# Strided and local attention with a rational MLP: row shape of the casts in memory, and queue order, PSUM banks and engine choices drawn anew

## The reference

```
scores = scale * q @ k^T                       # per batch and head
mask_local   = (rel >= 0) & (rel < 32)         # heads 0 to 3, rel = row - column
mask_strided = (rel >= 0) & (col % 32 == row % 32)   # heads 4 to 7
attn = exp(scores - max) / (sum + 1e-9), masked
x = (attn @ v), heads side by side             # 4608 x 512
h = x @ w_in                                   # 512 x 2048
P = a0 + a1*h + a2*h^2 + a3*h^3
Q = 1 + |b0|*|h| + |b1|*h^2
out = (P / (Q + 1e-6)) @ w_out                 # 2048 x 512
```

## Time and profile before

| | |
|---|---|
| three runs | 356.49, 356.37, 352.88 us; median 356.37 us |
| profiled execution | 355.32 us, of which the traced span is 353.5 us |
| busy in the span | PE 92%, DVE 91%, ACT 87%, POOL 21% |
| mean granted TensorE clock | 0.981 of full speed |

### The profile page before, as it was taken

One profiled execution on the slowest core, in us unless ns is written; L12 is line 12 of the kernel. 1 busy time (PEld: TensorE's weight loads), 2 busy tenths in 40 slices (PEclk: granted clock), 3 DMA queues, 4 the chain that ended last, 5 costly groups with the idle time before them and its releaser, 6 DMA issues.

```text
span 353.5 us, 9960 instructions
## 1 busy us (share of the span) xinstructions
PE 325.6 (92%) x4502; PEld 169.3 (48%) x4548; DVE 322.5 (91%) x282; ACT 307.1 (87%) x299; POOL 75.6 (21%) x112
## 2 busy tenths in 40 slices
PE   4979989999889998999999699999999999999796
PEld 1547667454444454455444354454444444444342
DVE  6573389999999999999999799999999999999995
ACT  6775389799998599999998798899999999999880
POOL 8980007060037043038003240000000000000000
PEclk9995799999999999999999999999999999999999
DMA  8999949999999999899699959510410011200203
GB/s 118 188 156 199 201 95 132 191 182 157 190 192 162 201 208 148 207 214 164 94 229 160 118 123 218 122 63 23 97 23 32 0 49 42 89 0 32 89 30 119
DMA packets 94314, 44.68 MB, mean 126 GB/s; under 512 B 79424, under 2 KB 87360, under 8 KB 93888
## 3 DMA queue, kind: packets, MB, share of 16 engines
q0 software_dynamic: 30528, 18.23, 42.1%
q1 hardware_dynamic: 63200, 25.69, 34.9%
q10 hardware_dynamic: 544, 0.13, 0.2%
HBM read 36.87 MB, written 16.52 MB: 151 GB/s over the span
## 4 chain that ended last, share of the span: by engine, by line
PE 60%; DVE 29%; ACT 6%; issue 4%; DVEq 0%
PE ps L1098 23%; PE ps L1168 22%; DVE h L1151 4%; DVE u L1126 4%; DVE z L1143 3%; DVE z L1147 3%; PE ps L683 3%; DVE u L1123 2%; DVE z L1140 2%; PE ps L1258 2%; DVE z L1149 2%; DVE z L1145 2%; ACT h L314 2%; DVE qkT L314 1%; PE ps L876 1%
## 5 line engine op out<-in xcount | busy, mean ns | idle before, releaser
L1168 PE MATMUL ps<-Wout,h 128*128 128x512 bf16 x543 | 129.2, 379 | 8.7 <-issue 5.9
L1098 PE MATMUL ps<-XT,Win 128*128 128x512 bf16 (+1 forms) x627 | 131.7, 361 | 4.9 <-issue 2.9
L1098 PEld LDWEIGHTS ps<-XT,Win 128*128 128x128 bf16 x640 | 61.5, 99 | 68.7 <-issue 4.0
L314 ACT ACTIVATE h<-ps 128x1024 bf16<-128x1024 f32 (+1 forms) x80 | 71.8, 958 | 16.6 <-PE ps L1098 16.6
L1168 PEld LDWEIGHTS ps<-Wout,h 128*128 128x128 bf16 x576 | 52.9, 98 | 63.7 <-issue 3.5
L1131 ACT ACTIVATE u<-u 128x4096 bf16<-128x4096 bf16 (+2 forms) x22 | 66.2, 3009 | 0.4 <-DVE u L1126 0.4
L1136 ACT ACTIVATE u<-u 128x4096 bf16<-128x4096 bf16 (+2 forms) x22 | 66.2, 3010 | 0.1
L1126 DVE TENSOR_TENSOR u<-u,z 128x4096 bf16<-128x4096 bf16 (+2 forms) x21 | 41.6, 1980 | 0.4
L1151 DVE TENSOR_TENSOR h<-z,u 128x4096 bf16<-128x4096 bf16 (+2 forms) x21 | 41.4, 1978 | 0.3
L1147 DVE TENSOR_TENSOR z<-z,h 128x4096 bf16<-128x4096 bf16 (+2 forms) x21 | 41.4, 1977 | 0.1
L1143 DVE TENSOR_TENSOR z<-z,h 128x4096 bf16<-128x4096 bf16 (+2 forms) x21 | 41.4, 1977 | 0.1
(11 more groups left out here) (106 smaller groups left out, 274.8 us busy)
## 6 DMA issues: line engine op xcount, KB each, us to landing
out_dram<-os SPq DMA_DIRECT2D x32, 256.0 KB, 2.5
qk<-in_k_dram POOLq DMA_DIRECT2D x12, 288.0 KB, 6.0
qk<-in_q_dram POOLq DMA_DIRECT2D x12, 288.0 KB, 6.1
Win<-in_moe_w_in_dram POOLq DMA_DIRECT2D x2, 1024.0 KB, 16.0
Wout<-in_moe_w_out_dram POOLq DMA_DIRECT2D x2, 1024.0 KB, 23.7
vS<-in_v_dram POOLq DMA_DIRECT2D x28, 72.0 KB, 5.8
vL<-in_v_dram POOLq DMA_DIRECT2D x28, 72.0 KB, 6.1
vL<-vL SPq DMA_DIRECT2D x14, 138.1 KB, 3.5
```

Of the source, the lines that this page charges most:

```text
L314: return lambda e: e.tensor_copy(o_(), i_()) if e_ == "dve" else e.activation(o_(), i_(), AF.Copy)
L1098: r = e.matmul(bank(ph, 512 * (s - s0) + n * i, n), Win[:, kk, f * 128:(f + 1) * 128], XT[:, kk, x0:x0 + n], start=(kk == 0), stop=(kk == ...
L1168: r = e.matmul(bank(po, 0, Fout), hf[:, j, m * 128:(m + 1) * 128], Wout[:, kk, :], start=(kk == 0), stop=(kk == NF - 1))
```

## The change

The casts' access patterns are written as 128 rows of 1152 elements instead of 16 rows of 9216, with another planner's cost. Four filler matmuls are added (`IDLE` 32 to 36). `SIDE`, `ORDER` and `AT` are all new.

```diff
@@ -446,11 +446,11 @@
     def bulk(b, nm, s_t, h0, slot, after):
         t = T_qk[nm, b]
         t.new()
-        n = HS // 16
+        n = HS // 128
         P.op("pool", lambda e: e.dma_start(
-            bass.AP(tensor=qk, offset=(4 * b + slot) * HS, ap=[[n, 16], [1, n]]),
-            bass.AP(tensor=s_t.tensor, offset=rows(s_t, b, h0), ap=[[n, 16], [1, n]])),
-            "issue", ("cast", b, nm), w=[t], dma=(16, 1380), after=after)
+            bass.AP(tensor=qk, offset=(4 * b + slot) * HS, ap=[[n, 128], [1, n]]),
+            bass.AP(tensor=s_t.tensor, offset=rows(s_t, b, h0), ap=[[n, 128], [1, n]])),
+            "issue", ("cast", b, nm), w=[t], dma=(128, 195), after=after)
...
-IDLE = 32
+IDLE = 36
 SIDE = (
-    "aaaddaadadadddaaadadaadaaaadaaaaadaaaaaaadadaadadaaaaaaddaddadaaaaaaddaaaaaadaaadadaaddaaaaaaaaaaaaa"
...
+    "daadadadaaaadadaaddddadadaaaaadadaaaaaddaaadadadaaaddddddadaaaaddadaddddaaaadaaadddaaddaaaaaaaaaaaaa"
...
 ORDER = {
     "pe": (
-        "1210 1229 1225 1211 1221 1206-1207 1230 1232 1224 63 1214 61 1226 1208 66-68 161 70 1203 1227 1204 "
...
+        "1225 1208 1234 1226 1231 1216 1232 1218 1215 1219-1220 63 61 1233 1236 1224 66-68 56 58 70 1206 1222 "
...
```

More of the change, by code:

```diff
@@ L1268 @@
 SIDE = (
-    "aaaddaadadadddaaadadaadaaaadaaaaadaaaaaaadadaadadaaaaaaddaddadaaaaaaddaaaaaadaaadadaaddaaaaaaaaaaaaa"
-    "aaaaddaaaaadaaaadaaaaaaaddaaaaaaaaaaaaaaaadaaaaaadaaaaaaaaaaadaaaaaadaaaaaaaaaaadaaaaaadaaaaaaaaaaaa"
-    "aaaaaadaaaaaaaaaaaaadaaaaaaaaaaaaddad"
+    "daadadadaaaadadaaddddadadaaaaadadaaaaaddaaadadadaaaddddddadaaaaddadaddddaaaadaaadddaaddaaaaaaaaaaaaa"
+    "aaaadddaaaaaaaaaaaaaaaadddaaaaaaaaaaaaaaaadaaaaaadaaaaaaaaaaaaaaaaaadaaaaaaaaaaadaaaaaadaaaaaaaaaaad"
+    "aaaaaadaaaaaaaaaaaaaaaaaaaaaaaaaaaadd"
 )
@@ L1338 @@
 AT = (
-    "3675705660245071135021272720374561660304317117206032455247254405005125066073500020220404423140631433"
-    "4620016644035144612126046246574745615662040646060751206101641420556341241124513313136473042620465124"
-    "4107522470633360042005017627122772402"
+    "1754500741153050067233777212510325060775164037066465145010432260530510532723203027602304664423306046"
+    "5666620440510030557522020246701205242466616201674016325234320461601427451533354626421465155003570730"
+    "76037016406252502274546211130324755113260"
 )
```

## The result

The changed kernel takes **352.51 us** (median of 20 runs, 349.6 to 356.87) where the kernel before takes 356.55 us in as many runs (352.88 to 361.68): ratio 0.9888, interval 0.9861 to 0.9915. So it is faster by 0.6 to 1.1%, 2 to 4 us, which is at the border of what the prediction called no change: its border for faster was 352.8 us, and the two medians are 352.51 and 353.26. The ratios compare those runs of a kernel that lie within 1.5% of its fastest; of e2's twelve runs five took 360.8 to 367.0 us and are left out by this.

The account below looks back on a forecast made before the run. The start-up chain was taken to bound the kernel up to the first u1, then DVE's work plus few waits. 3.2 - 1.9 + 0 - 0.4 = +0.9 on 355.32 gave 356.2 us; own range 353.5 to 359, whole range 350.5 to 361.5.

Parts of the forecast that it names:

- R1: Rival at the start up to W1: TensorE keeps its higher clock, -5.0 us, giving 351.2; chance 0.32.
- Casts: Casts in POOL's queue: the new row shape makes the same transfer and costs nothing, 0 us.
- R3: Rival on the casts: the row shape takes effect, 16 rows become 128 a cast, time stays 356.2; chance 0.03.
- A: Start of the first u1: 10.98 us behind W1's start, +3.2 us, at about 46.3; bounds nothing and +5.2.
- B: DVE's work from u1 to the last g: -1.9 us, all of it on the path.
- C: DVE's waits after u1: taken as equal, 0; bounds -2.9 and +4.4 us.
- D: Tail after the last g: ten rather than twelve W2 matmuls depend on it, -0.4 us.
- R2: Rival on ACT up to ex of group (6,0): two |h| make it late, DVE waits, +3.6 us, 359.8; chance 0.20.

Follow-up runs that it names:

- e2: Changed kernel's operations up to the first u1, then all others in the order of the kernel before: ratio 0.9987 to the kernel before.
- e8: Changed kernel with casts that really go in 128 pieces of 2.3 KB: ratio 0.9893 to the kernel before.
- e10: Kernel before with casts that really go in 128 pieces of 2.3 KB, nothing else changed: ratio 1.0008 to the kernel before.
- e4: Changed kernel with SP's three small constants' loads ahead of its first vL transfers, as before: ratio 0.9856 to the kernel before.
- e7: Changed kernel without the seven filler matmuls ahead of the first W1: ratio 0.9933 to the kernel before.
- e11: Changed kernel with casts of 128 real pieces and the constants loaded ahead of vL's transfers: ratio 0.9939 to the kernel before.
- e12: Changed kernel with 32 pairs of neighbours in DVE's queue exchanged, for more dependent neighbours: 359.25 us, ratio 1.0114 to the kernel before.
- e6: Kernel before with the |h| of groups (3,0), (3,1) and (9,0) moved to ACT: 369.17 us, ratio 1.0344 to the kernel before.
- e1: Order of the kernel before for what the first u1 needs, then the changed kernel's for the rest: ratio 0.9985 to the kernel before.
- e5: Order of the kernel before up to the first g, then the changed kernel's for the rest: ratio 1.0043 to the kernel before.

## Why the prediction was right and where it was not

The time lay in the whole range, 350.5 to 361.5, 3.7 us under the forecast, and a change of about 1% was foreseen as what can hardly be told from none. But the sum had the wrong sign, +0.9 for the -2 to -4 that the ratios stand for, and 352.51 lies below the forecast's own range of 353.5 to 359. The whole range reached it only because it had been drawn to take in R1, which is not what happened; so far it was luck. What the sum said of the middle was too little.

- **Casts and R3: right.** Same shape, same packets, and no effect even where the pieces are real (e8, e10). The rule that R3 took from the Trainium skill ("DMA: Bandwidth & Descriptors", Rules for kernel authors) is stated there for a tile in SBUF; for these casts, from memory to memory, the 30528 packets decide against it.
- **A, start of the first u1: right in size.** +3.2 was forecast; +1.55 and +4.06 were measured, 11.14 and 10.67 behind W1 for 10.98. That W1's own start stayed where it was, on which the 46.3 rests, did not hold: it moved by -1.84 and +1.14, and in four more profiles with this order, but for their edits, u1 stands at 44.92 to 48.32 (e4, e7, e8, e11). That the two measured values lie around +3.2 is so far luck; the 10.98 behind W1 is not. The wait for constants was overlooked, an SP queue that the prediction had not followed; e4 shows that it costs nothing measurable.
- **B, DVE's work: mis-sized.** -1.9 was forecast and -3.8 measured. The counted moves came out as counted. What was left out is that 48 dependent neighbours became 36: 12 x 0.08 = 1.0 of busy time and 12 x 0.04 = 0.5 of gaps. About 0.9 more lies in the scalings (u1, p1, p3, p5). About 0.5 of that comes from those right behind a reciprocal, 0.09 to 0.10 shorter behind L656 in four places and 0.05 to 0.09 behind L1023 in four, where the kernel before has two; most of the rest is three single scalings of before that took 0.10 to 0.17 longer than the others of their line, and why stays open. The prediction took each instruction's duration from the rows and let the overlaps be the same; a new order changes just them. e12 shows the term of the dependent neighbours. The work is also what stays: in all six profiles with the changed kernel's order in the middle (with e4, e7, e8 and e11) DVE is busy for 293.5 to 293.9 us, for 297.2 and 297.3 in the two with the order of before (with e10).
- **C, waits: mis-sized.** 0 was forecast with -2.9 as the lower bound. Waits over 0.25 us were 3.6 us in all before (of which 2.9 in the earlier trace rows) and 1.6 in the changed kernel; the rest of the fall of idle time from 6.43 to 3.20 is gaps below that. But this does not belong to the new order as the work does: its six profiles have 2.75, 3.20, 3.52, 4.83, 7.82 and 8.20 of idle time, the larger ones with a PE stall at L876, and the two with the order of before 6.04 and 6.43. That the new order has fewer waits in most runs is not shown.
- **D, tail: right in sign.** Ten matmuls follow the end of the last g, as forecast, and the gain is 0.2 for 0.4 (by the prediction's own price, two matmuls at 0.235, it should have said 0.5).
- **R1 is not what made it faster.** The granted clock stayed up longer in both profiles of the changed kernel, but also in e10 with the order of before, and not in e4. W1 ran its first pieces at 1.90 for 8 matmuls, the lower level, and its last at 1.05, the upper, and u1 was later than before. Without the fillers no other time was found (e7). R1's price also misread a row: the 5.80 us of W1 before are not all at the lower level, since the clock rose at 39.39, inside them, so that 0.66 is not the ratio of the levels.
- **R2 did not happen, and was the right danger.** No wait for ex appears; in the old order the same moves cost 12 us (e6). Its account was off in two places. The two |h| stand ahead of 130 us, where ACT had 7.3 us to spare; and where ACT does become late, in e6, DVE waits most at u1 for |h| itself, 5.5 us, which R2 did not look at, and 3.5 at g for ex. In the changed kernel DVE waits 0.7 us at u1. What in the new order keeps ACT in time was not tested by itself.

By the two profiles the sum is: start +1.6 to +4.1, middle -7.0 to -7.5, tail -0.2, which is -3.6 to -5.7 against the profile of before. The measured ratios stand for -2 to -4. What can be relied on is DVE's shorter work in the middle, 3.4 to 3.8 us, against a start that is later by 1.6 us or more; the idle time varies from run to run by more than the whole gain. Why e1 and e5, which have the shorter work too, are no faster than before is not settled.

## What to carry to other kernels

On an engine that sets the time, count beside the durations how many instructions stand right behind one that they depend on; taking turns between two independent chains was worth 0.12 us a place here. A move between engines has no price of its own: the same three moves gained about 2% in an order drawn for them and cost 3.4% in one that was not. One profile of a kernel whose runs differ by 2% doesn't show which waits belong to it, and here two did not either: six were needed to see that the work belonged to the order and the waits did not.

## What the runs showed of the hardware

- A DVE instruction that depends on the one right before it began about 0.04 us after its end, most others about 0.08 before it: 46 of the 48 dependent neighbours in the profile of before and 34 of the 36 in each profile of the changed kernel, the others 0.08 to 0.10 after it. The Trainium skill, "Perfetto Trace Analysis", section DVE / Act Engine Instruction, says that the recorded end is the acknowledged write and that the semaphore is seen after it; the kernel orders its own engine's dependent instructions by semaphores, and the 0.04 agrees.
- A scaling of 128x4096 on DVE right behind a reciprocal is recorded shorter: 1.18 to 1.19 us behind L656 in all four cases of both profiles of the changed kernel, 1.27 to 1.29 elsewhere at L1145 and L1149. No run tells why.
- PE stalls with no visible cause ("issue") of over 1 us came in every profile, at places that vary from run to run of the same order. Eleven of the 14 profiles have one of 1.9 to 4.1 us at L604 or L683 shortly ahead of W1, seven have one of 1.4 to 4.6 us at L876 about 135 us, and the granted clock fell beside some of them. In e4:

```profile
133.15 0.26 PE L876 MATMUL ps<-qkT 64*18 64x18 bf16 x25 [1.74 <-issue]
...
133.70 6.09 PE L1168 MATMUL ps<-Wout,h 128*128 128x512 bf16 x20
```
```profile
133.15:139.60 6.45, 6.45 (x50) 2.87 (x50) 6.45 (x6) 3.45 (x3) 3.47 (x3) 0.74 1.20 179
```

The granted clock is 0.74 there. In the changed kernel's first profile the same matmuls went without a stall, 19 of them in 4.26 us. The cause of the stalls stays open.
